# A scan and expert kernel on one core: three tile shapes a step in the scan, other places for the weight loads and for u, and c^T turned in the last step

## The reference, cut to what matters

```python
# 1: a linear-attention scan; B, H, S, D = 4, 8, 768, 48
for t in range(S):
    cur = einsum('bhd,bhe->bhde', u * k[t], v[t])
    y[t] = einsum('bhd,bhde->bhe', r[t], state + cur)
    state = w * state + einsum('bhd,bhe->bhde', k[t], v[t])
# 2: soft mixture of experts; x = y as 3072 tokens x 384, 8 experts x 4 slots, F = 1024
logits = x @ phi
d = softmax(logits, over tokens); slot_input = d.T @ x
slot_out[e] = relu(slot_input[e] @ w1[e]) @ w2[e]
c = softmax(logits, over slots);  x = c @ slot_out
# 3: feed-forward 384 -> 2048 -> 384
h = x @ w_in
out = (h * sigmoid(1.702 * h)) @ w_out
```

## Time and profile before

| | us |
|---|---|
| median of three runs (386.47, 387.59, 392.37) | 387.59 |
| the profiled execution | 386.26 |
| its span, first to last instruction | 384.5 |
| PE busy in the span (3220 records) | 373.3 |
| DVE, ACT, POOL busy | 234.3, 186.2, 96.4 |
| moved by DMA, in MB | 63.76 |

### The profile page before, as it was taken

The page is one execution under the profiler, slowest core; times in us unless marked ns, Lnnn a source line. Parts: engine busy times, 40 slices in busy tenths (PEclk is TensorE's granted clock), DMA queues, the critical chain, the costliest instruction groups (busy, mean ns, idle before and its releaser), DMA issues.

```text
span 384.5 us, 9081 instructions
## 1 busy us (share of the span) xinstructions
PE 373.3 (97%) x3220; PEld 292.9 (76%) x3220; DVE 234.3 (61%) x429; ACT 186.2 (48%) x410; POOL 96.4 (25%) x113
## 2 busy tenths in 40 slices
PE   7799999999999999999999999999999999999996
PEld 6678787887876344568888888888888888888885
DVE  6787878887784301678756555655565556655660
ACT  1235454545434441576564456445644464465552
POOL 5888788787672110000000000000000000000000
PEclk9999999999999999999999999999999999999999
DMA  7899999999999899700001002000200020002002
GB/s 231 292 328 396 397 389 398 388 363 368 401 356 414 349 377 413 274 0 3 0 27 57 0 2 82 0 0 0 82 0 0 0 82 0 0 0 82 0 2 82
DMA packets 21797, 63.76 MB, mean 166 GB/s; under 512 B 3088, under 2 KB 6816, under 8 KB 21392
## 3 DMA queue, kind: packets, MB, share of 16 engines
q1 hardware_dynamic: 20432, 62.99, 43.2%
q10 hardware_dynamic: 1344, 0.49, 0.7%
HBM read 58.75 MB, written 4.72 MB: 165 GB/s over the span
## 4 chain that ended last, share of the span: by engine, by line
PE 92%; POOL 3%; DVE 1%; issue 1%; ACT 1%; DMA 1%; DVEq 0%; POOLq 0%; ACTq 0%
PE bank L588 11%; PE bank L589 11%; PE bank L587 11%; PE bank L347 6%; PE pair L587 6%; PE pair L386 6%; PE pair L589 5%; PE pair L588 5%; PE bank L572 4%; PE pair L377 3%; PE pair L369 3%; PE bank L407 3%; PE bank L534 3%; PE bank L514 2%; PE bank L334 2%; PE bank L398 2%
## 5 line engine op out<-in xcount | busy, mean ns | idle before, releaser
L855 DVE TENSOR_TENSOR gf<-bank,sg 128x512 f32<-128x512 f32 x72 | 49.7, 691 | 59.1 <-ACT sg L1050 58.8
L1050 ACT ACTIVATE sg<-bank 128x512 f32<-128x512 f32 x72 | 42.9, 597 | 73.5 <-PE bank L572 73.5
L588 PE MATMUL bank<-ghi,whi 128*128 128x512 f32 x190 | 73.9, 389 | 0.0
L587 PE MATMUL bank<-glo,whi 128*128 128x512 f32 x190 | 73.9, 389 | 0.0
L589 PE MATMUL bank<-ghi,wlo 128*128 128x512 f32 x190 | 73.9, 389 | 0.0
L861 DVE TENSOR_TENSOR glo<-gf,ghi 128x512 fp32r<-128x512 f32 x96 | 66.3, 691 | 1.0 <-ACT ghi L1056 0.7
L1056 ACT ACTIVATE ghi<-gf 128x512 fp32r<-128x512 f32 x96 | 60.0, 625 | 2.0 <-DVE gf L855 1.9
L938 ACT ACTIVATE yt<-pair 112x512 f32<-112x512 f32 x24 | 14.3, 598 | 56.5 <-PE pair L386 56.5
L587 PEld LDWEIGHTS bank<-glo,whi 128*128 128x128 f32 x190 | 35.7, 188 | 7.4
L589 PEld LDWEIGHTS bank<-ghi,wlo 128*128 128x128 f32 x190 | 35.7, 188 | 7.4
L588 PEld LDWEIGHTS bank<-ghi,whi 128*128 128x128 f32 x190 | 35.7, 188 | 7.4
(11 more groups left out here) (176 smaller groups left out, 516.5 us busy)
## 6 DMA issues: line engine op xcount, KB each, us to landing
ring<-w SPq DMA_DIRECT2D x24, 512.0 KB, 6.2
rkb<-rk SPq DMA_DIRECT2D x23, 512.0 KB, 5.3
krb<-kr SPq DMA_DIRECT2D x24, 384.0 KB, 5.4
ring<-w SPq DMA_DIRECT2D x4, 1536.0 KB, 13.3
ring<-w SPq DMA_DIRECT2D x8, 768.0 KB, 8.9
vb<-v SPq DMA_DIRECT2D x24, 192.0 KB, 5.5
out<-ob SPq DMA_DIRECT2D x18, 256.0 KB, 2.1
ring<-win SPq DMA_DIRECT2D x3, 1024.0 KB, 14.7
```

The source lines that it names most:

```text
L587: pe.matmul(o, w_hi, lo, start=(f == 0), stop=False)
L588: pe.matmul(o, w_hi, hi, start=False, stop=False)
L855: dve.tensor_tensor(gf[:, f % 2, :], bank[f % 4][:, :], sg[:, f % 2, :], ALU.mult).then_inc(gf_ok, 1)
L1050: act.activation(sg[:, f % 2, :], bank[f % 4][:, :], ACT.Sigmoid, scale=1.702).then_inc(sg_ok, 1)
```

## The change

- **TensorE.** The scores are computed in sixteen matmuls with 64 output rows each (64x64 tiles) where there were eight. `outputs` is cut into `bonus_turns` (the four transposes), `earlier` (the part of the earlier state) and `outputs` (scores times v). From chunk 1 on a step runs `earlier(n-1)`, `scores(n)`, `outputs(n-1)`, `state(n-1)`, `tokens(n-2)`, `bonus_turns(n)`: the transposes of step n come behind the tokens' in step n, where they were in step n + 1. A semaphore `vd_used` tells of them. `gather` follows `bonus_turns`. 10 warm-up matmuls stand at the start where 17 were, 7 where 4 were.
- **VectorE.** `scale(n+1)` stands ahead of `mask(n)` from chunk 1 on, slot maxima and row sums stand elsewhere in their steps. In chunk 0 VectorE multiplies by u, which GpSimd did. The table of powers at the start is chained operation by operation.
- **ScalarE.** `decay` stands ahead of `columns`; three constants are loaded by SP after the first step of chunk 1, and phi behind the first copy.
- **SP.** The first loads are in another order. Chunk 1 has three pieces of w1 (five before), chunks 2 to 4 five each as before, chunk 5 six (2, 2, 1, 1; four before).
- **Last step.** `turned_weights(1)` stands in step 23, ahead of `bonus_turns(23)`, and waits for `c_ok` there; GpSimd's product that gives `c_ok` stands ahead of its `vd`. Behind the scan the spreads, logits and slot inputs are in another order.

```diff
+HALVES = (slice(0, 64), slice(64, P))
-WARM = 17
+WARM = 10
...
+            load_rk(0, 0)
+            load_kr(0, 0)
+            load_rk(0, 1)
+            load_v(0, 0)
+            load_kr(0, 1)
+            load_v(0, 1)
+            step(0, 2, 0, 0)
+            step(0, 3, 0, 0)
+            step(1, 0, 0, 0)
+            for dst, src in ((same[:, :], match), (jcol[:, :], jsel), (pick[:, :, :], sel)):
+                sp.dma_start(dst, src).then_inc(s_late, 16)
+            step(1, 1, 0, 0)
+            step(1, 2, 0, 1)
+            step(1, 3, 1, 2)
+            with sp.Fori(2, C - 1) as c:
+                for b in range(B):
+                    step(c, b, (B + 1) * (c - 2) + 3 + b, 1 if b < B - 1 else 2)
+            step(C - 1, 0, 18, 2)
+            step(C - 1, 1, 20, 2)
+            step(C - 1, 2, 22, 1)
+            step(C - 1, 3, 23, 1)
...
                 for hp in range(HP):
-                    for p0, i in HEADS:
-                        s = slice(p0, p0 + D)
-                        last = pe.matmul(SC[i][:, hp * CH:(hp + 1) * CH],
-                                         rks[s, b % 2, 1, hp, :], rks[s, b % 2, 0, hp, :], start=True, stop=True)
+                    for half in HALVES:
+                        for p0, i in HEADS:
+                            s = slice(p0, p0 + D)
+                            last = pe.matmul(SC[i][half, hp * CH:(hp + 1) * CH],
+                                             rks[s, b % 2, 1, hp, half], rks[s, b % 2, 0, hp, :], start=True, stop=True)
...
+                if not is_first(c, b):
+                    earlier(*prev(c, b))
                 scores(c, b)
                 if not is_first(c, b):
+                    if is_first(c):
+                        bonus_turns(*prev(c, b))
                     outputs(*prev(c, b))
...
+                if is_last(c) and b == B - 1:
+                    pe.wait_ge(s_new, B * (C - 1) + 1)
+                    pe.wait_ge(c_ok, 1)
+                    turned_weights(1, 0, 4)
+                if not is_first(c) or b == B - 1:
+                    bonus_turns(c, b)
+                if tail and b == 2:
+                    gather(c - 1, LG, 2 * c)
...
             outputs(C - 1, B - 1)
             tokens(C - 1, B - 2)
-            pe.wait_ge(c_ok, 1)
-            turned_weights(1, 0, 4)
-            logits(C - 1)
-            tokens(C - 1, B - 1)
-
-            pe.wait_ge(s_late, 16 * 3)
             pe.wait_ge(own_ok, 2 * B)
             pe.wait_ge(clo_ok, 1)
             spread_weights(1)
+            logits(C - 1)
+            tokens(C - 1, B - 1)
+            spread_weights(2)
...
+                if is_first(c):
+                    dve.wait_ge(rk_ok, n + 1)
+                    if b == 0:
+                        dve.wait_ge(s_const, 16 * 2)
+                    dve.tensor_tensor(rkn[:, b % 2, :, :], rkn[:, b % 2, :, :], ubc[:, :, :], ALU.mult)\
+                       .then_inc(rku_ok, 1)
                 dve.wait_ge(rku_ok, n + 1)
...
+                if is_first(c) and b:
+                    mask(c, b)
+                    scale(*following(c, b))
+                else:
+                    if more:
+                        scale(*following(c, b))
+                    mask(c, b)
...
+                if is_last(c) and b == 3:
+                    pool.wait_ge(rsum_ok, 1)
+                    pool.tensor_tensor(*row_terms(1, 0, EARLY), ALU.mult).then_inc(c_ok, 1)
                 bonus_values(c, b)
```

More of the change, by code:

```diff
@@ L270, in step, with load_v, load_w1 @@
                 sp.dma_start(krb[:, b % 2, :, :, :], kr_v[n]).then_inc(kr_in[b % 2], 16)
+            def load_v(c, b):
+                n = B * c + b
                 wait(sp, st_ps, n - 3)
                 sp.dma_start(vb[:, b, :, :], v_v[n]).then_inc(v_in[b], 16)
[L275 to L278, removed]
+            def load_w1(first, count):
+                for i in range(count):
+                    sp.dma_start(ring_flat[:, bass.ds((first + i) * FE, FE)], w1_v[first + i]).then_inc(w1_in, 16)
+            def step(c, b, first, count):
+                load_rk(c, b)
+                load_kr(c, b)
+                load_v(c, b)
+                load_w1(first, count)
+            load_rk(0, 0)
[19 more added lines that the diff above has]
+            step(C - 1, 3, 23, 1)
             def w2_slot(e):
@@ L355, in scores, with bonus_turns @@
                     last.then_inc(wkn_ps, 1)
-                    keep_warm(LG, 4)
-            def outputs(c, b):
+                    keep_warm(LG, 7)
+            def bonus_turns(c, b):
                 n = B * c + b
-                if not is_first(c):
-                    wait(pe, s_new, n - 2)
                 wait(pe, yt_ok, n)
@@ L372, in outputs, with earlier @@
                                          skip_group_check=True)
-                if not is_first(c):
+                last.then_inc(vd_used, 1)
+            def earlier(c, b):
+                n = B * c + b
+                if is_first(c):
+                    pe.sem_inc(rs_used, 1)
+                else:
+                    wait(pe, s_new, n - 2)
+                    pe.sem_inc(tiles_go, 1)
                     for a in range(2):
@@ L380, in outputs @@
                                                  start=False, stop=False, skip_group_check=True)
-                last.then_inc(rs_used, 1)
+                    last.then_inc(rs_used, 1)
+            def outputs(c, b):
+                n = B * c + b
                 wait(pe, masked, 2 * n + 2)
@@ L432, in gather, with turned_weights @@
                 last.then_inc(p_ps, 1)
+            def turned_weights(which, c0, c1):
+                for c in range(c0, c1):
+                    last = pe.transpose(bank[TURN[which]][:, (c - c0) * P:(c - c0 + 1) * P],
+                                        lnat[:, c, :, :].rearrange("p b s -> p (b s)"), idt[:, :])
+                last.then_inc(cturn_ps, 1)
             def step(c, b):
@@ L501, in _ @@
             last.then_inc(si_ps, 1)
-            spread_weights(0)
             pe.wait_ge(si_ok, 1)
@@ L789, in step @@
-                bonus_sum(c, b)
+                more = not (is_last(c) and b == B - 1)
                 if tail and b == 1:
                     slot_max(c - 1)
+                if is_first(c) and b:
+                    mask(c, b)
+                    scale(*following(c, b))
+                else:
+                    if more:
+                        scale(*following(c, b))
+                    mask(c, b)
+                if is_last(c) and b == 2:
+                    row_sum(*early)
+                if more:
+                    bonus_sum(*following(c, b))
```

151 lines of the change are left out of this document (73 added, 78 removed).

## The result

| | before | changed |
|---|---|---|
| median, us | 387.26 (20 runs) | 389.19 (20 runs, 386.96 to 391.07) |
| ratio | | 1.0050, 95% interval 1.0035 to 1.0064 |
| profiled execution, us (its span) | 386.26 (384.5) | 389.24 (387.3) |
| first expert layer begins | 127.99 | 130.81 |
| mean granted clock of that execution | 0.999 | 0.991 |

Forecast were 382.0 us in a range of 378.6 to 386.3, so this is a miss of 7 us on the wrong side. The span grew by 2.8 us, and the first expert layer starts 2.8 us later: as foreseen, all of the difference arises ahead of it.

A forecast was written before the change was run, and what follows sets the result against it. PE was taken to set the scan's pace, with transfers close behind. Gains of 1.9, 1.25 and 2.55 us, less 2.7 for late pieces, left the feed-forward 4.5 earlier: 381.8, forecast as 382.0 us, range 378.6 to 386.3.

The forecast's parts named there:

- the 0.3 that `wout` was to cost: Ahead of the feed-forward: first quarter of wout lands at 152.0 for a use at 151.7, 0.3 us lost.
- A step of the scan: PE's loop: three tile shape changes instead of five save 0.28 us a step; halved scores keep their 0.91 us.
- The transfers of a chunk: Chunks 2 to 4: 7.08 MB take 17.8 us, so PE's 17.5 is not reached; 0.85 won each, 2.55 together.
- The rival with 0.15: Chunks 2 to 4: transfers keep PE's pace, 3.45 us won instead of 2.55, total 379.3 us; chance 0.15.
- Chunk 1 "PE sets it at 17.5": Chunk 1: with two w1 pieces less, transfers need 15.4 us, so PE sets 17.5 and 1.25 is won.
- The two late pieces: Last chunk: two w1 pieces moved from chunk 1 cost 2.7 us, leaving transfers 3.0 ahead of a 5.7 lead.
- The start: Chunk 0: seven warm-up matmuls less start the first scores at 7.39, 1.9 us won; chunk 1 begins at 23.9.
- The last chunk: Step 23: last krb lands at 109.3, POOL's chain makes vd ready at 113.5, last outputs start at 114.6, 4.8 ahead.
- The rival with 0.06: Step 23: bonus_turns waits for krb and 4.2 us of POOL, deciding from a landing at 114.0; 387.9 us, chance 0.06.
- the sign that was named: Last step: PE waits one to three us ahead of the last bonus_turns, ended by vd.
- Behind the scan: Last outputs to first expert layer: transposes gone (0.5 us), slot-input copy open (about 0.6), nothing in sum.
- The clock "is no term here": Scan chunks: granted clock 1.00, the 2.4 GHz level, in all windows, so no time was set for it.

The follow-up runs named there:

- before_small_scores: The kernel before with only the scores in 64x64 tiles (sixteen matmuls), at their old place: 388.04 us, ratio 1.0022.
- full_scores: The changed kernel with the scores in eight matmuls of 128 output rows again: 387.45 us, ratio 1.0015 to the kernel before.
- early_thinned: The changed kernel with five w1 pieces in every chunk from the second on, plus one 48x512 matmul a step ahead of the scores: 408.99 us, two runs.
- before_w1_late: The kernel before with only SP's list of w1 pieces taken from the changed kernel: 389.36 us, ratio 1.0051.

## Why the prediction was wrong

From its own marks the forecast goes wrong as follows: chunk 1 begins 2.7 us later than forecast (26.59 for 23.9, of which 1.16 are the new order alone), takes 4.8 longer, chunks 2 to 4 take 0.5 less, and from the start of chunk 5 to outputs(23) it takes 1.0 longer (20.8 for 19.8). That makes 8.0 at outputs(23). From there to the expert layer it is 0.3 better than forecast, and the 0.3 that `wout` was to cost did not come: 7.4, the miss of the profiled execution.

- **A step of the scan: right.** 3.91 us a step for 3.88, halved scores at the price of whole ones; 3.0 won in chunks 2 to 4.
- **The transfers of a chunk: wrong, in the good direction.** 17.8 us was forecast from a rate of 401 GB/s; 404 in the window of chunk 3 carries 7.08 MB in 17.5. The rate seen before was PE's demand, and the slice of 401 (96 to 106 us) lies half behind the loop. The rival with 0.15 had this term right.
- **Chunk 1 "PE sets it at 17.5": this step failed, by 4.8 us.** I reckoned PE's groups at their loop prices and no price for the first time through the code. The hole of 2.63 and the stretch at half clock are most of it (in that stretch three groups take 1.5 us more from start to start than in chunk 3). before_small_scores, full_scores and early_thinned show that the hole belongs to a dense instruction stream in the first pass.
- **The two late pieces, 2.7 us out of a lead of 5.7: this step failed too.** I counted the bytes left out of chunk 1 as room for nothing ("a chunk with 2 us of room"), and charged 2.7 us to the last chunk, to be paid out of a lead of 5.7. The lead was never there (chunk 1 had a share of 0.91 where 1.03 is full, and PE was late), so the debt fell due in full: the last two `rkb` and `krb` land 3.6 to 4.3 us later than before. before_w1_late measures it alone: 2.1 us.
- **The start: mis-sized, and compared at the wrong point.** The first scores came at 7.90 (forecast 7.39), but chunk 0 took 18.7 us; less the 1.16, that is 4.4 a step and not 3.9 (4.1 before). And I set the fifth scores against 25.77, though the new order puts 1.16 us of groups ahead of them: 26.93 is the like point. Won: 0.3 of 1.9. Why chunk 0 is longer stays open; the kernels with u on GpSimd took 17.9 to 19.3 for it, so it is not u alone.
- **The last chunk: the chain was right in part, its input wrong.** The rival with 0.06 ("the last step turns into the bound") comes nearest to what came: last `krb` at 116.1, beyond its threshold of 114.0, + 5.4 = 121.5, and outputs(23) at 122.57. The 1.1 between them is mostly POOL's wait of 0.98 for the row sums (`rm`), which DVE made late. And the sign that was named, a wait of one to three us ended by `vd`, did not come: it was 0.16. PE had lost its time at scores(23) already, by way of `rkb`, scale(23) and mask(22), a path that the prediction does not have. I gave it 0.06 because it "needs both other terms to fail"; they failed together, since both rested on chunk 1.
- **Behind the scan: right in kind.** The same path runs from outputs(23) to the expert layer; the copy of the slot inputs stands open by 0.35 (forecast 0.6).
- **The clock "is no term here": wrong.** In the runs of the changed kernel the three executions at a mean clock of 1.00 took 387.7 us on average, the eight at 0.996 took 388.4, the four at 0.991 took 389.6. Each stretch of 3.4 us at the 1.2 GHz level goes with about 1 us; whether it costs this or the gap ahead of it does, the times alone do not tell. In the traces ten such stretches begin 0.5 to 1.6 us behind the end of a gap of PE of 1.66 to 3.15 us; six gaps of 1.66 to 2.48 us had none behind them.

## What to carry to other kernels

Before judging a transfer as deferred for free, ask which later stretch has to carry it and whether its lead is already measured or only forecast: two pieces of w1 moved out of a stretch that had carried them at no cost into a later one that was full cost 2.1 us by themselves. Price the first pass of a loop apart from the later ones: an order that is denser in instructions can win in every pass and lose as much in the first. Terms that rest on the same stretch (here chunk 1) fail together, and a rival that "needs both to fail" deserves more than the product of their chances.

## What the runs showed of the hardware

- TensorE stopped for up to 3.15 us in the middle of a group, one to three times in the first pass of a loop and in the straight code behind it, and each time went on 2.3 to 2.8 us after a 16,384-byte instruction transfer of 1.0 to 1.4 us had begun. In the first pass of the loop it stopped so with 43 to 45 records a us and not with 35 to 36. How far ahead the blocks are asked for, and why it needs 1.3 to 1.6 us behind the landing, stays open.
- A semaphore increment as an instruction of its own took TensorE 0.15 us where nothing hid it (64 more of them moved its first matmul by 9.8 us, and the whole by 8.1 to 8.6).
- One core's transfers ran at 404 GB/s over whole chunks of 17.5 us. The Trainium skill (DMA: Bandwidth & Descriptors, Bandwidth) has about 358 GB/s a core as the limit from HBM, and says that each core gets about this when both of a pair stream; this program ran on one core, and the measurement is above it.
